# Attention and MLPs on one core: transposes and ranking one step later, and every second product with v moved out by ScalarE and added by GpSimd

## The chip, the cores and the metric

The kernel runs on one NeuronCore of a Trainium2 chip. The metric is the device time of one execution in microseconds, the median of several. Engines are named as in the profile: PE is TensorE (PEld its weight loads), DVE is VectorE, ACT is ScalarE, POOL is GpSimd, and SP issues most DMAs.

## What is computed

All in float32, and three stages in a row:

```
q_assign, k_assign = argmax over 16 centroids of the normalised q and k (per head)
scores = q @ k.T / 8, masked where q_assign != k_assign      16 heads of 768 x 64
x = softmax(scores) @ v                                      1536 tokens x 512
x = rational(x @ moe_w_in) @ moe_w_out                       d_ff 2048, P(h)/Q(h) elementwise
out = (silu(x @ w_gate) * (x @ w_val)) @ moe2_w_out          d_ff 1536
```

## The kernel before, in words

To keep float32 accuracy every operand is split into a high and a low part, so that a product is two or three matmuls (`three`, L1107 on; the names end in `_hi` and `_lo`). Each engine has its own program, written out in one block per engine, and they meet by semaphores.

The attention is a loop over `STEPS`. Step `s` holds the scores of tile `s` (96 tiles: 16 heads, 6 tiles of 128 queries each), and, so many steps behind, what follows for earlier tiles. On each engine the parts of a step run in the order in which they are written:

- PE: scores of tile `s` (L1226, L1229) into one of two double banks; transposes of the probabilities of tile `s - LAG` (L1239) into the two banks at `PT_BANK`, once DVE has read the tile before; a third of a product with v (L1254, L1256) into `O_BANK`; then, in some steps, the ranking's transposes (L1278), ranking (L1292) and centroid logits (L1313) of a head to come.
- DVE: cluster rows (L1024, L1026), `neg_max` of tile `s` (L1035), in steps divisible by 3 the row sums and reciprocals (L1046, L1049), `probT_lo` of tile `s - LAG` in two halves (L1057), `x_raw` (L1066), logit sum and maximum (L1072, L1074), `is_top` (L1080).
- ACT: exp of tile `s - 1` (L811), `topT` (L819), `probT_hi` in two halves (L829), `x_part` (L839), `logit_lo` (L861).
- POOL: normalising three tiles every third step (L589), splitting a head's q and k (L597 to L606) in steps divisible by 6, v (L614, L617) three steps later, the first MLP's weights (L624, L626), and every fourth product the x pair (L636, L638).

A product `g` is half a head: 384 query columns, summed over three steps. It begins `PV_LAG = LAG + 3` steps behind. Its result in `O_BANK` is two halves of 64 rows, which must be added: ACT copies one out to `x_part`, DVE adds the other to it into `x_raw`. The next product waits for that, since there is one bank. POOL splits `x_raw` of two heads into `x_hi` and `x_lo`, `X_STEP` steps behind.

The preparation of a head `h` (split, logits, sum, top, transposes, ranking, cluster rows: the stages `S_SPLIT` to `S_CLUSTER`) is placed by `head_at`, 18 steps ahead of the head's scores, and its rows go by SP's queue as small DMAs (`send_cluster`, L390) into `qk_low`, which the first score of the head waits for.

The first MLP begins inside the loop: PE makes the hidden values of tiles 0 to 3 in pieces in steps 96 to 103 (`TAIL_CHUNKS`), and ACT, DVE and POOL do tile 0 in step 98 and tile 1 in step 100 (`TAIL`; `hidden_read`, `mlps`, `mlp1`), ACT its second part in steps 99 and 101 (`TAIL_LOG`; `hidden_finish`). `mlps(1)` has six instructions of DVE (L925 to L953), and its last waits for `g_hi` of ACT's step 101. After the loop `first_result(0)` uses `O_BANK` and so waits for the last extraction. POOL's part of tile 2 (L516) stands behind the last x pair.

```
def pv_at(step):
    g, third = (step - PV_LAG) // HALF, (step - PV_LAG) % HALF
    return (g, third) if 0 <= g < NG else (None, None)
```

## Time and profile before

| | |
|---|---|
| runs | 794.30, 794.31, 795.95 us, median 794.31 |
| profiled execution | 794.28 us, its span 792.5 us |
| busy in the span | PE 781.2 (99%), PEld 697.7, DVE 571.9, ACT 517.3, POOL 522.7 us |
| HBM | 46 GB/s over the span |
| attention loop | 0 to about 263 us: x_part 32 times, from 37.0 to 262.2 us |

Rows of a timeline are: start in us from the span's start, duration, engine, line, operation, output<-inputs, shapes, count, and in brackets how long the engine sat idle before and what ended that. The end of a matmul is modelled, so that PE reads as busy in parts of its waits; the starts are measured.

### The profile page before, as it was taken

The numbers are of one execution on the slowest core, as the hardware profiler recorded it, in microseconds if no ns is written. First come the engines' busy times: TensorE is split into PE (matmuls) and PEld (weight loads), VectorE is DVE, ScalarE is ACT, GpSimd is POOL, SyncE is SP. The second block draws the span as 40 slices with busy tenths as digits, with TensorE's granted clock in tenths as the row PEclk, the third lists the DMA queues.
The fourth block names the chain that finished last, engine by engine and source line by source line (L and its number), as shares of the span: only waits on it lengthen the run. The fifth ranks groups of instructions, "written<-read, shape, count | busy, mean of one in ns | idle before, by whom it ended". The sixth has DMA issues, their size and how long they took to land.

```text
span 792.5 us, 12617 instructions
## 1 busy us (share of the span) xinstructions
PE 781.2 (99%) x4204; PEld 697.7 (88%) x4204; DVE 571.9 (72%) x1043; ACT 517.3 (65%) x957; POOL 522.7 (66%) x457
## 2 busy tenths in 40 slices
PE   8999999999999999999999999999999999999998
PEld 7799999999998888888888888899999999999997
DVE  5899999999997888778777777745445545554453
ACT  4888888888887787777767889744444444333322
POOL 4767988998575799322222288888889876655620
PEclk8999999999999999999999999999999999999999
DMA  8776555454310700000000011241111114111102
GB/s 206 180 199 162 143 140 125 116 145 121 85 60 19 221 28 0 1 1 1 1 1 0 1 55 54 66 147 50 32 54 53 37 45 134 54 28 53 28 1 80
DMA packets 57681, 57.92 MB, mean 73 GB/s; under 512 B 6608, under 2 KB 44304, under 8 KB 57616
## 3 DMA queue, kind: packets, MB, share of 16 engines
q1 hardware_dynamic: 57376, 56.52, 26.6%
q8 instruction: 34, 0.56, 0.3%
q10 hardware_dynamic: 240, 0.59, 0.3%
q14 instruction: 31, 0.25, 0.1%
HBM read 33.59 MB, written 3.15 MB: 46 GB/s over the span
## 4 chain that ended last, share of the span: by engine, by line
PE 87%; DVE 8%; issue 2%; ACT 2%; DMA 0%; DVEq 0%; ACTq 0%
PE ps L1111 18%; PE ps L1109 18%; PE ps L1110 18%; PE ps L1239 6%; PE ps L1204 4%; PE ps L1205 4%; PE ps L1203 4%; DVE neg_max L1035 3%; DVE probT_lo L1057 3%; PE ps L1254 3%; PE ps L1226 3%; PE ps L1256 3%; PE ps L1313 2%; PE ps L1229 2%; ACT prob L811 1%
## 5 line engine op out<-in xcount | busy, mean ns | idle before, releaser
L516 POOL TENSOR_TENSOR den<-den,mag 128x512 f32<-128x512 f32 x48 | 62.3, 1298 | 121.8 <-ACT den L689 121.6
L1111 PE MATMUL ps<-x_hi,w_lo 128*128 128x512 f32 (+1 forms) x384 | 139.5, 363 | 0.0
L1109 PE MATMUL ps<-x_hi,w_hi 128*128 128x512 f32 (+1 forms) x384 | 139.4, 363 | 0.0
L1110 PE MATMUL ps<-x_lo,w_hi 128*128 128x512 f32 (+1 forms) x384 | 139.3, 363 | 0.0
L575 POOL TENSOR_TENSOR w_lo<-w_raw,w_hi 128x768 fp32r<-128x768 f32 (+1 forms) x48 | 101.6, 2125 | 56.4 <-ACT w_hi L742 56.4
L589 POOL TENSOR_SCALAR prob<-prob,row_inv 128x768 f32<-128x768 f32 x96 | 85.6, 907 | 39.2 <-DVE row_inv L1049 38.7
L829 ACT ACTIVATE probT_hi<-ps 128x384 fp32r<-128x384 f32 x192 | 84.2, 489 | 25.9 <-PE ps L1239 24.2
L1057 DVE TENSOR_TENSOR probT_lo<-ps,probT_hi 128x384 fp32r<-128x384 f32 x192 | 96.8, 545 | 5.3 <-ACT probT_hi L829 4.0
L1035 DVE TENSOR_REDUCE neg_max<-ps 128x1 f32<-128x768 f32 x96 | 91.1, 950 | 8.8 <-PE ps L1229 8.5
L811 ACT ACTIVATE prob<-ps,neg_max 128x768 f32<-128x768 f32 x96 | 86.8, 905 | 10.8 <-DVE neg_max L1035 10.1
L1239 PE MATMUL ps<-ident,prob 128*128 128x128 f32 x576 | 81.7, 277 | 4.4 <-DVE probT_lo L1057 4.1
L1239 PEld LDWEIGHTS ps<-ident,prob 128*128 128x128 f32 x576 | 65.6, 140 | 17.0 <-issue 9.9
L1109 PEld LDWEIGHTS ps<-x_hi,w_hi 128*128 128x128 f32 x384 | 72.1, 188 | 8.2
L1110 PEld LDWEIGHTS ps<-x_lo,w_hi 128*128 128x128 f32 x384 | 72.1, 188 | 8.2
L1111 PEld LDWEIGHTS ps<-x_hi,w_lo 128*128 128x128 f32 x384 | 72.1, 188 | 7.5
L1111 PE MATMUL ps<-g_hi,w_lo 128*128 128x512 f32 x192 | 74.8, 390 | 0.0
L1110 PE MATMUL ps<-g_lo,w_hi 128*128 128x512 f32 x192 | 74.8, 390 | 0.0
L1109 PE MATMUL ps<-g_hi,w_hi 128*128 128x512 f32 x192 | 74.8, 390 | 0.0
L1254 PE MATMUL ps<-probT_hi,v_split 128*128 128x384 f32 x192 | 72.5, 378 | 0.0
L763 ACT ACTIVATE act_hi<-ps 128x384 fp32r<-128x384 f32 x48 | 23.6, 492 | 64.6 <-DVE ps L992 43.7
L1256 PE MATMUL ps<-probT_lo,v_split 128*128 128x384 f32 x192 | 64.6, 337 | 0.0
L959 DVE TENSOR_TENSOR sum<-ps,gate 128x384 f32<-128x384 f32 x24 | 13.4, 557 | 68.9 <-PE ps L1111 68.9
(145 smaller groups left out, 1987.5 us busy)
## 6 DMA issues: line engine op xcount, KB each, us to landing
k_hihi<-qk_hi SPq DMA_DIRECT2D x32, 192.0 KB, 4.0
w_raw<-in_moe_w_gate SPq DMA_DIRECT2D x48, 128.0 KB, 2.3
w_raw<-in_moe_w_val SPq DMA_DIRECT2D x48, 128.0 KB, 2.5
w_raw<-in_moe_w_in SPq DMA_DIRECT2D x16, 256.0 KB, 3.7
w_raw<-in_moe_w_out SPq DMA_DIRECT2D x16, 256.0 KB, 5.0
qk_raw<-in_q SPq DMA_DIRECT2D x16, 192.0 KB, 3.4
q_hilo<-qk_hi SPq DMA_DIRECT2D x16, 192.0 KB, 3.4
qk_low<-qk_hi SPq DMA_DIRECT2D x16, 192.0 KB, 4.5
```

Of the source, the lines that this page charges most:

```text
L575: did(g.tensor_tensor(lo[:, wave, :], raw[:, wave, :], hi[:, wave, :].bitcast(F32), ALU.subtract), s_w2lo)
L589: did(g.tensor_scalar(prob[i][:, :], prob[i][:, :], row_inv[:, i:i + 1], 1.0, ALU.mult, ALU.mult), s_norm)
L811: s.activation(prob[i % T][:, :].rearrange("p (c n) -> p c n", c=2), ps[:, bank:bank + 2, 0:HC], ACT.Exp, bias=neg_max[:, i % T:i % T + 1] ...
L829: s.activation(probT_hi[g % 2][:, n * HALF:(n + 1) * HALF, c:c + P], ps[:, PT_BANK + n, 0:HC].rearrange("p (k n) -> p k n", k=HALF), ACT.C ...
L1035: v_.tensor_reduce(neg_max[:, i % T:i % T + 1], ps[:, bank:bank + 2, 0:HC], AX.XY, ALU.max, negate=True).then_inc(s_max, 1)
L1057: v_.tensor_tensor(probT_lo[g % 2][:, keys, c:c + P], ps[:, PT_BANK + n, 0:HC].rearrange("p (k n) -> p k n", k=HALF), probT_hi[g % 2][:, k ...
L1109: mm(dst, hi, m_hi, start=start, stop=False)
L1110: mm(dst, hi, m_lo, start=False, stop=False)
L1111: return mm(dst, lo, m_hi, start=False, stop=stop)
L1239: last = transpose(ps[:, PT_BANK + n, kt % HALF * P:(kt % HALF + 1) * P], prob[i % T][:, kt * P:(kt + 1) * P], ident[:, :])
L1254: mm(ps[:, O_BANK, 0:HC], vv, probT_hi[g % 2][:, kt, :], start=(kt == 0), stop=False)
L1256: last = mm(ps[:, O_BANK, 0:HC], vv, probT_lo[g % 2][:, kt, :], start=False, stop=(kt == T - 1))
```

## The change

`LAG` goes from 5 to 6, so transposes, `probT_hi`, `probT_lo` and the products come one step later. The preparation stages from the logits on come one step later for heads 2 and up (head 2 had this already up to its sum). The x pairs of POOL follow their product by 1 step instead of 5 (the last one by 2).

The extraction of a product depends on its number now. Even ones go as before. For odd ones ACT copies both halves, one into `x_raw` and one into `x_low`, a tile that lies where `x_hi` will, DVE does nothing, and POOL adds the two (384 columns of both heads of a pair in one instruction) ahead of the split. PE waits for `s_xsum` or `s_xmain` by turns.

```
--- before.py
+++ after.py
@@ -85,6 +85,7 @@
     x_hi = at("x_hi", [P, DC, NTOK], F32R, X_AT)
     x_lo = at("x_lo", [P, DC, NTOK], F32R, X_AT + X_BYTES)
 
+    x_low = at("x_low", [P, DC, NTOK], F32, X_AT)
     x_raw = at("x_raw", [P, DC, NTOK], F32, X_AT + X_BYTES)
 
     w1_raw = [at(f"w1_raw{u}", [P, U1], F32, W_AT + u * 8 * U1) for u in range(NF1)]
@@ -218,8 +219,8 @@
     s_cen_in, s_par_in = sem("s_cen_in"), sem("s_par_in")
     s_qk_in = [sem(f"s_qk_in{i}") for i in range(3)]
     s_v_in = [sem(f"s_v_in{i}") for i in range(2)]
-    s_vhi, s_vlo, s_logit_lo, s_logit_sum, s_xpart, s_xsum = (sem(x) for x in (
-        "s_vhi", "s_vlo", "s_logit_lo", "s_logit_sum", "s_xpart", "s_xsum"))
+    s_vhi, s_vlo, s_logit_lo, s_logit_sum, s_xpart, s_xsum, s_xmain = (sem(x) for x in (
+        "s_vhi", "s_vlo", "s_logit_lo", "s_logit_sum", "s_xpart", "s_xsum", "s_xmain"))
     s_copy = [sem(f"s_copy{i}") for i in range(3)]
     s_clrows = [sem(f"s_clrows{i}") for i in range(3)]
     s_w1_in = [sem(f"s_w1_in{u}") for u in range(NF1)]
@@ -237,6 +238,7 @@
         "s_score", "s_max", "s_exp", "s_den", "s_inv", "s_norm"))
     s_pT, s_pT_hi, s_pT_lo, s_pv, s_xhi, s_xlo = (sem(x) for x in (
         "s_pT", "s_pT_hi", "s_pT_lo", "s_pv", "s_xhi", "s_xlo"))
+    s_xboth = sem("s_xboth")
     s_w1p_hi, s_w1p, s_w1hi, s_w1lo = (sem(x) for x in ("s_w1p_hi", "s_w1p", "s_w1hi", "s_w1lo"))
     s_w2sum, s_w2hi, s_w2lo, s_wohi, s_wolo = (sem(x) for x in (
         "s_w2sum", "s_w2hi", "s_w2lo", "s_wohi", "s_wolo"))
@@ -254,10 +256,10 @@
 
     R_LAG = 3
     COPIES, CLROWS = 16 * 6, 16 * T
-    LAG = 5
+    LAG = 6
     PV_LAG = LAG + HALF
     V_STEP = 3
-    X_STEP, LAST_X_STEP = 5, 2
+    X_STEP = 1
     PREP_LEAD = 18
     FIRST_STEP = -PREP_LEAD
     S_SPLIT, S_CEN, S_LOGIT, S_SUM, S_TOP, S_TOPT, S_RANK, S_CLUSTER = 0, 2, 6, 8, 9, 10, 11, 12
@@ -269,7 +271,9 @@
 
 
         for h in range(NH):
-            late = -4 * (h == 1) + (h == 2 and stage <= S_SUM)
+            late = -4 * (h == 1)
+            if h >= 2:
+                late = 1 if stage >= S_LOGIT else int(h == 2)
             if T * h + late == step + PREP_LEAD - stage:
                 return h
         return None
@@ -626,13 +630,14 @@
                     did(g.tensor_tensor(w1_lo[u][:, :], w1_raw[u][:, :], w1_hi[u][:, :].bitcast(F32),
                                     ALU.subtract), s_w1p)
                 g1, third = pv_at(step - X_STEP)
-                if pv_at(step - LAST_X_STEP) == (NG - 1, HALF - 1):
-                    g1, third = NG - 1, HALF - 1
                 if third == HALF - 1 and g1 % 4 == 3:
-                    pool.wait_ge(s_xsum, g1 + 1)
+                    h = g1 // 2
+                    pool.wait_ge(s_xmain, h + 1)
+                    pool.wait_ge(s_xsum, h + 1)
                     finish_last()
-                    h = g1 // 2
                     xh, xl, raw = x_pair(x_hi, h), x_pair(x_lo, h), x_pair(x_raw, h)
+                    did(g.tensor_tensor(raw[:, HC:S], raw[:, HC:S], x_pair(x_low, h)[:, HC:S], ALU.add), s_xboth)
+                    finish_last()
                     did(g.tensor_scalar(xh, raw, 1.0, 1.0, ALU.mult, ALU.mult), s_xhi)
                     pool.wait_ge(s_xhi, h // 2 + 1)
                     did(g.tensor_tensor(xl, raw, xh.bitcast(F32), ALU.subtract), s_xlo)
@@ -834,10 +839,14 @@
                 if third == HALF - 1:
                     r = (g // 2) % 2 * D
                     sc.wait_ge(s_pv, g + 1)
-                    if g:
-                        sc.wait_ge(s_xsum, g)
-                    s.activation(x_part[r:r + D, :], ps[D - r:P - r, O_BANK, 0:HC], ACT.Copy
-                                 ).then_inc(s_xpart, 1)
+                    if g % 2 == 0:
+                        if g:
+                            sc.wait_ge(s_xsum, g // 2)
+                        s.activation(x_part[r:r + D, :], ps[D - r:P - r, O_BANK, 0:HC], ACT.Copy
+                                     ).then_inc(s_xpart, 1)
+                    else:
+                        s.activation(x_of(x_low, g), ps[D - r:P - r, O_BANK, 0:HC], ACT.Copy)
+                        s.activation(x_of(x_raw, g), ps[r:r + D, O_BANK, 0:HC], ACT.Copy).then_inc(s_xmain, 1)
                 if head_at(step, S_CEN) == 0:
 
                     sc.wait_ge(s_cen_t, 4)
@@ -1059,9 +1068,9 @@
                                          probT_hi[g % 2][:, keys, c:c + P].bitcast(F32),
                                          ALU.subtract).then_inc(s_pT_lo, 1)
                 g, third = pv_at(step)
-                if third == HALF - 1:
-
-                    ve.wait_ge(s_xpart, g + 1)
+                if third == HALF - 1 and g % 2 == 0:
+
+                    ve.wait_ge(s_xpart, g // 2 + 1)
                     r = (g // 2) % 2 * D
                     v_.tensor_tensor(x_of(x_raw, g), ps[r:r + D, O_BANK, 0:HC],
                                      x_part[r:r + D, :], ALU.add).then_inc(s_xsum, 1)
@@ -1142,7 +1151,8 @@
                 pe.wait_ge(s_glo, n + 1)
                 if n == 0:
                     pe.wait_ge(s_pT_lo, 2 * NT)
-                    pe.wait_ge(s_xsum, NG)
+                    pe.wait_ge(s_xsum, NH)
+                    pe.wait_ge(s_xmain, NH)
                 for d in range(DC):
                     if u == 0 and n:
                         pe.wait_ge(s_yraw, (n // NF1 - 1) * DC + d + 1)
@@ -1248,7 +1258,7 @@
                         pe.wait_ge(s_pT_lo, T * (g + 1))
                         pe.wait_ge(s_vlo, h + 1)
                         if g:
-                            pe.wait_ge(s_xsum, g)
+                            pe.wait_ge(s_xsum if g % 2 else s_xmain, (g + 1) // 2)
                     for kt in (2 * third, 2 * third + 1):
                         vv = v_split[h % 2][:, kt, :, :].rearrange("p two d -> p (two d)")
                         mm(ps[:, O_BANK, 0:HC], vv, probT_hi[g % 2][:, kt, :], start=(kt == 0),
```

## Rows read from the trace of the kernel before

**Rows 1.** Busy time by stretch: span, then PE, PEld, DVE, ACT, POOL, clock, DMA.
```profile
46.80:213.00 166.20, 162.75 (x1116) 153.17 (x1114) 157.78 (x334) 138.84 (x317) 139.21 (x139) 1.00 0.54 135
213.00:243.00 30.00, 29.45 (x192) 26.95 (x189) 29.46 (x57) 26.73 (x61) 22.72 (x24) 1.00 0.15 46
...
263.40:520.00 256.60, 256.60 (x1142) 213.71 (x1142) 197.73 (x289) 196.76 (x303) 140.24 (x101) 1.00 0.10 30
```

**Rows 2.** What PE waited for, whole span: us in total, times, longest.
```profile
PE ps L1239 <- DVE probT_lo L1057: 4.1, 14, 0.5
```

**Rows 3.** One head, DVE in order of time: start, us, line, operation.
```profile
134.25 0.96 DVE L1035 TENSOR_REDUCE neg_max<-ps 128x1 f32<-128x768 f32 x1 [0.31 <-PE ps L1229]
...
136.05 0.36 DVE L1072 TENSOR_TENSOR ps<-ps,logit_lo 128x192 f32<-128x192 f32 x1
...
137.58 0.15 DVE L1046 TENSOR_REDUCE row_den<-row_sum 128x3 f32<-128x6 f32 x1
...
140.93 0.56 DVE L1066 TENSOR_TENSOR x_raw<-ps,x_part 64x384 f32<-64x384 f32 x1
...
142.51 1.02 DVE L1057 TENSOR_TENSOR probT_lo<-ps,probT_hi 128x384 fp32r<-128x384 f32 x2
```

**Rows 4.** The same head, PE.
```profile
138.53 0.92 PE L1239 MATMUL ps<-ident,prob 128*128 128x128 f32 x6 [0.21 <-DVE probT_lo L1057]
...
141.64 0.41 PE L1254 MATMUL ps<-probT_hi,v_split 128*128 128x384 f32 x1
```

**Rows 5.** The same head, ACT.
```profile
132.87 0.49 ACT L839 ACTIVATE x_part<-ps 64x384 f32<-64x384 f32 x1 [0.16 <-PE ps L1256]
133.38 0.90 ACT L811 ACTIVATE prob<-ps,neg_max 128x768 f32<-128x768 f32 x1
...
134.58 0.88 ACT L829 ACTIVATE probT_hi<-ps 128x384 fp32r<-128x384 f32 x2 [0.20 <-PE ps L1239]
```

**Rows 6.** Groups by line, 0 to 300 us: a two-input operation of POOL.
```profile
L617 POOL TENSOR_TENSOR v_split<-v_raw,v_split 128x384 fp32r<-128x384 f32 x16 | 16.2, 1013 | 1.3
```

**Rows 7.** The last two cluster-row DMAs of head 2, their landing, and PE's next score.
```profile
L390 SPq DMA_DIRECT2D qk_low<-clusterT x2: 592/593/594, 36.4 to 37.1; - x2
...
DMA to landing us min/median/max: 1.9/2.0/2.1
...
39.20 0.52 PE L1226 MATMUL ps<-k_hihi,q_hilo 128*128 128x384 f32 x2
```

**Rows 8.** End of attention, ACT.
```profile
247.45 0.49 ACT L839 ACTIVATE x_part<-ps 64x384 f32<-64x384 f32 x1 [0.16 <-PE ps L1256]
...
249.92 0.61 ACT L685 ACTIVATE mag<-ps 128x512 f32<-128x512 f32 x1
...
262.18 0.48 ACT L839 ACTIVATE x_part<-ps 64x384 f32<-64x384 f32 x1 [0.98 <-PE ps L1256]
```

**Rows 9.** End of attention, DVE.
```profile
252.07 0.69 DVE L944 TENSOR_TENSOR num<-num,ps 128x512 f32<-128x512 f32 x1 [1.36 <-ACT num L693]
...
253.46 1.01 DVE L1057 TENSOR_TENSOR probT_lo<-ps,probT_hi 128x384 fp32r<-128x384 f32 x2
...
256.92 0.69 DVE L925 SCALAR_TENSOR_TENSOR den<-den,ps 128x512 f32<-128x512 f32 x1
...
260.42 0.68 DVE L953 TENSOR_TENSOR g_lo<-ps,g_hi 128x512 fp32r<-128x512 f32 x1
```

**Rows 10.** End of attention, PE.
```profile
251.39 0.82 PE L1239 MATMUL ps<-ident,prob 128*128 128x128 f32 x6
...
254.15 0.92 PE L1239 MATMUL ps<-ident,prob 128*128 128x128 f32 x6
...
257.04 0.41 PE L1254 MATMUL ps<-probT_hi,v_split 128*128 128x384 f32 x1
...
263.41 0.47 PE L1109 MATMUL ps<-g_hi,w_hi 128*128 128x512 f32 x1
```

**Rows 11.** End of attention, POOL.
```profile
266.20 1.29 POOL L516 TENSOR_TENSOR den<-den,mag 128x512 f32<-128x512 f32 x1
```

More of the change, by code:

```diff
@@ L256, in build_program @@
     COPIES, CLROWS = 16 * 6, 16 * T
-    LAG = 5
+    LAG = 6
     PV_LAG = LAG + HALF
     V_STEP = 3
-    X_STEP, LAST_X_STEP = 5, 2
+    X_STEP = 1
     PREP_LEAD = 18
@@ L271, in head_at @@
         for h in range(NH):
-            late = -4 * (h == 1) + (h == 2 and stage <= S_SUM)
+            late = -4 * (h == 1)
+            if h >= 2:
+                late = 1 if stage >= S_LOGIT else int(h == 2)
             if T * h + late == step + PREP_LEAD - stage:
@@ L1061, in _ @@
                 g, third = pv_at(step)
-                if third == HALF - 1:
-                    ve.wait_ge(s_xpart, g + 1)
+                if third == HALF - 1 and g % 2 == 0:
+                    ve.wait_ge(s_xpart, g // 2 + 1)
                     r = (g // 2) % 2 * D
```

32 lines of the change are left out of this document (20 added, 12 removed).

## Prediction

> **What bounds the kernel now.** I read the busy times by stretch first. In the MLPs TensorE is busy for all of 256.6 us out of 256.6 [rows 1], so a microsecond lost ahead of them is not won back there; the end moves by as much. In the attention loop four engines are near full: from 46.8 to 213 us PE 162.8, DVE 157.8, ACT and POOL 139 of 166.2 us [rows 1]. Which of PE and DVE sets the pace is read from PE's waits: only one kind recurs, the transposes of L1239 waiting for probT_lo, 14 times, 4.1 us in all, at most 0.5 [rows 2]. So PE sets the pace, with about one stop per head of 6 steps. The busy PE records hide part of each (their ends are modelled), so I take 0.53, near the longest, rather than the mean of 0.3: 0.38 at the transposes and 0.15 at a product (both below). A lighter DVE can then return at most 0.53 x 13 = 6.9 us in the loop, for the 13 heads prepared in it.
>
> **Where the stop per head comes from.** DVE meets PE at 134.25, where neg_max has waited for its score [rows 3]. From there DVE works without a pause: logit sum and maximum (136.05), row sums and reciprocal (137.58), is_top, three neg_max, three pairs of probT_lo, and at 140.93 x_raw of the even product, which ends at 141.49 [rows 3]. PE is stopped by this chain twice [rows 4]: the transposes at 138.53 waited for probT_lo (0.21 by the row, nearer 0.4 by the starts around it), and the product at 141.64 begins 0.15 after x_raw ended; it needs the same bank.
>
> **The change in the loop.** Three things move by one step together: the transposes (LAG), the ranking stages from the logits on, and with LAG the products. Relative to each other they stand as before: the logit sum is still two steps ahead of the even product's extraction. What is removed is x_raw of the odd product. It lies one step ahead of the logit sum, beside two long steps of PE with logits, and DVE has 0.31 us idle behind it before 134.25 [rows 3]. Taking it away makes that idle time longer; the chain from 134.25 to 141.49 keeps every member, for the row sums (steps divisible by 3, not moved) are in it once before and once after. **Removed DVE work, 16 instructions of 0.55 us: worth 0 in these heads.**
>
> The row sums of the second half do move against the rest. They stood in a long logit step; now they follow the even extraction directly, in the short step with the ranking. There x_raw ends at 141.49, one neg_max of 0.96 follows, and probT_lo starts at 142.51 [rows 3], which leaves nothing between them. Row sums and reciprocal add 0.27 (0.15 for the first and about as much for the second), less the 0.1 by which neighbours on DVE overlap: probT_lo 0.15 later, and the next transposes with it; in heads where probT_lo waits for ACT anyway, about 0.04. **I take 0.1 x 13 = +1.3 us; bounds 0 and 2.3.**
>
> ScalarE gets a second copy of 0.49 us per head. Before, x_part at 132.87 is followed by exp at 133.38 and probT_hi at 134.58, 0.2 us after the engine was free [rows 5]. Two like copies take 0.88, so they start 0.4 apart [rows 5]; exp moves by 0.42, and the first probT_hi runs from 134.8 to 135.3 instead of to 135.07. DVE is through with neg_max at 135.1 to 135.2 [rows 3]; but the row sums now stand ahead of probT_lo in just this step, so DVE comes at 135.39. Hidden, with 0.03 us to spare: **0, bounds 0 and 1.3.** If that cover were gone the price would be a rival below. For PE the bank comes free after 2 copies (0.9) instead of copy plus x_raw (1.1): 0.
>
> GpSimd adds 8 two-input operations on 128x384, each 1.01 as its like [rows 6], 8.1 us into 139.2 busy of 166.2 [rows 1]. The x pair moves from the step with a head's split to the one with v_split, the smaller of the two, and the norms have one step more before their transposes. SP's queue waits on GpSimd's v_split, which still stands ahead of the x pair: 0. The GpSimd page of the Trainium skill (GPSIMD Engine Reference, section Engine selection) says to keep elementwise adds off this engine, at about twice the vector engine's time. Here 1.01 against 0.55 bears out the ratio; were they on the path that ends last, the 8 adds would cost 3.7 us by it, which I do not count since POOL has that time.
>
> **The start.** With transposes one step later, PE and DVE have less to do ahead of step 12: one step's transposes and one step's products, about 1.4 us of PE (a step without extras is some 2.1: a third each for scores, transposes and products, and two of these three are missing once). But step 12 opens head 2, whose cluster rows are sent by SP. The last two go out at 36.4 and 37.1 and land 1.9 to 2.1 us later, at 39.2, and the score starts at 39.20 [rows 7]. SP issues them one after another behind other copies of the same queue, whose own conditions the change leaves alone, so they come no earlier. PE is ready 1.4 sooner, at about 37.8, and waits. **Start: +0.1 us; the 1.4 us of work that left here is lost, as it comes back at the end.** Bounds -1.3 (the rows are not what ends it) and +0.3.
>
> **The last steps with scores** (213 to 243 us): no ranking, short steps, DVE busy 29.5 of 30.0 [rows 1]. Here a dropped x_raw helps; but the two copies of ACT now delay exp and so probT_hi, about 0.5 us in each of 2 places, and step 96 waits 0.2 more since the even extraction falls just before it. **0, bounds -1.0 and +0.9.**
>
> **The end of attention: the main term.** The MLP's first two tiles are begun at steps 98 and 100 (TAIL), and these did not move with LAG. Each engine runs its steps in order.
> (a) Step 98: ACT now first does the two copies of product 29 (before: nothing). Its last copy of this kind was at 247.45 and a step is 254.15-251.39 = 2.76 us [rows 8, 10], so they start at 250.2 and end at 251.1; mag of tile 0 moves from 249.92 [rows 8] to 251.1, 1.2 later. DVE's num (252.07) waits for it, probT_lo (253.46) stands behind num [rows 9], and the transposes at 254.15 start 0.15 after its first half ended [rows 10]: no slack. **+1.2 us.**
> (b) Step 100: DVE does tile 1's six instructions, from 256.92 to 261.10 [rows 9], 4.2 us. Before, the last probT_lo and x_raw of product 30 stood ahead of them and PE's product at 257.04 followed at once. Now both are of step 101, behind them. With (a), the transposes of step 100 are at 255.4, the probT_lo of that step ends 2.1 later at 257.5, the block runs to 261.7, then probT_lo 0.93 and x_raw 0.56 to 263.2, 0.15 to PE: 263.3. PE is through with step 101 at 255.4 + 2 x 2.76 = 260.9. **+2.3 us.**
> (c) The last product is now at step 104, behind the last chunk. Before, x_part (262.18) and x_raw ran beside the chunk of step 103 and first_result began at 263.41 [rows 8, 10]. Now nothing covers 0.2 + 2 copies 0.9 + 0.15. **+1.2 us.**
> (d) The extra step's transposes and products, 1.3 us, are the work that left the start. **+1.3 us.**
> GpSimd's last pair takes 1.0 longer, which moves den at 266.20 [rows 11] by 1.0 against PE; tile 2's g_lo then comes about 0.1 ahead of its use: 0, at most 0.3.
> Together +6.0; bounds 3.5 and 7.5.
>
> **Sum.** 0.1 + 1.3 + 0 + 6.0 = 7.4 us on the profiled execution's 794.28, whose span is 792.5; that execution is within 0.03 of the median 794.31. Forecast **801.6**; its own range, with the ends of the terms not all at once, 798 to 804.5.
>
> **Rivals.**
> *Faster: DVE is the true bound.* Busy 95% in the loop [rows 1], it stops PE 14 times [rows 2]. If the stops go in all 13 heads (-6.9), the row sums cost nothing, the start keeps its work (-1.3) and the last scores gain (-1.0), the time is 794.3+6.0-9.2 = 791.1, give or take 2. Against it: the chain of rows 3 loses no member. A rule of the Trainium skill (Perfetto Trace Analysis, Identifying the Most-Contended Engine) judges TensorE's room by weight-load time. That is 153.2 of 166.2 us here [rows 1], 13 us of room against the 4 to 7 that the waits allow; by it the time could come to 781, and it has 0.02 of this rival's chance. Chance 0.14, of it 0.04 within the bound of no change.
> *No change.* The end is absorbed: (a) and (b) overlap with other slack, and only 1 to 2 us stay, against a small gain in the loop: 793 to 796. For it: DVE has idle time there, 1.36 us ahead of 252.07 [rows 9]. Chance 0.07.
> *Slower still: ACT's second copy is not covered.* It decides from 0.03 us of lateness of probT_hi in the step of rows 5. If DVE would be there at once, probT_hi holds it by the whole 0.42: 0.4 x 13 = 5.2 on top, 806.8. Chance 0.07.
> *The change doesn't do what it says.* The bank's waits are split over two semaphores and each product has its own; I see no case where the old path stays. 0.
> Forecast: 0.72.
>
> **Numbers.** A difference under 0.2% (1.6 us) can't be told from no change. Forecast and last rival give slower, 0.79, and 0.01 of the no-change case does, 0.8 together; same is 0.04 of that case and 0.04 of the faster one, 0.08; faster is the rest, 0.12. The range 796.5 to 804.5 holds the forecast's range and 1.5 us towards no change, where most of what I may have overrated at the end would put it.
>
> **What would show it.** Right: the waits of L1239 for probT_lo still about 13, of 0.3 to 0.6, a step later; x_raw of DVE 16 times with an idle DVE where the other 16 were; PE gaps near 254, 261 and 268 us of about 1.2, 2.3 and 1.2; first_result's start at 269 to 271 instead of 263.41; PE busy without gaps behind it. PE's clock stays at its 2.4 GHz level, as in the stretches of rows 1. Wrong: fewer than 6 waits of L1239 on probT_lo, the score of step 12 before 38.5, or no PE gap over 1 us between 250 and 275.

## The result, and the profile after

The kernel with the change took 802.84 us (median of 6 runs, 801.08 to 803.57) beside 795.13 us for the kernel before (794.23 to 797.3) on the same chip. The ratio is 1.009, with a 95% interval of 1.0071 to 1.0108: slower by 0.9%. The forecast was 801.6, within 796.5 to 804.5.

The profiled execution took 801.45 us, 7.17 more than before; its span is 799.7. Busy time by stretch, same columns as [rows 1]:

```profile
46.14:213.00 166.86, 164.89 (x1114) 152.52 (x1114) 149.51 (x320) 142.26 (x329) 144.23 (x144) 1.00 0.53 135
```

DVE has 8.3 us less to do in the loop (157.8 to 149.5), ACT 3.4 and POOL 5.0 more. The loop is not shorter. What DVE did with its 8 us stands in one group of the kernel after, columns as in [rows 6] (the last part is the idle time ahead of the group):

```profile
L1044 DVE TENSOR_REDUCE neg_max<-ps 128x1 f32<-128x768 f32 x96 | 91.2, 951 | 20.4 <-PE ps L1239 20.0
```

and in the same group of the kernel before:

```profile
L1035 DVE TENSOR_REDUCE neg_max<-ps 128x1 f32<-128x768 f32 x96 | 91.1, 950 | 8.8 <-PE ps L1229 8.5
```

The window is 0 to 300 us. DVE waits 11.6 us longer ahead of `neg_max`: the removed additions became idle time there. x_raw itself is down to 16 additions from 32.

**Where the 7 us are.** PE's first matmul of a step is the score; here is that of steps 0, 6 and 81 before (step 12 is in [rows 7]), and of steps 0, 6, 12 and 81 after:

```profile
15.62 0.56 PE L1226 MATMUL ps<-k_hihi,q_hilo 128*128 128x384 f32 x2
...
25.28 0.51 PE L1226 MATMUL ps<-k_hihi,q_hilo 128*128 128x384 f32 x2
...
209.07 0.51 PE L1226 MATMUL ps<-k_hihi,q_hilo 128*128 128x384 f32 x2
```

```profile
15.54 0.56 PE L1236 MATMUL ps<-k_hihi,q_hilo 128*128 128x384 f32 x2
...
24.32 0.59 PE L1236 MATMUL ps<-k_hihi,q_hilo 128*128 128x384 f32 x2 [0.42 <-ACT prob L816]
...
38.48 0.59 PE L1236 MATMUL ps<-k_hihi,q_hilo 128*128 128x384 f32 x2 [0.69 <-issue]
...
209.56 0.60 PE L1236 MATMUL ps<-k_hihi,q_hilo 128*128 128x384 f32 x2
...
270.53 0.47 PE L1118 MATMUL ps<-g_hi,w_hi 128*128 128x512 f32 x1 [1.16 <-ACT x_raw L849]
```

The last row is `first_result`, which was at 263.41 [rows 10]. The stretches between such starts make the table that the rest of this text uses (us; "steps 39 to 75" are six heads from the middle of the loop, six times a steady head):

| kernel (profiled execution) | step 0 at | 0 to 6 | 6 to 12 | 12 to 27 | 27 to 81 | of it 39 to 75 | 81 to 95 | median of runs |
|---|---|---|---|---|---|---|---|---|
| before | 15.62 | 9.66 | 13.93 | 37.11 | 132.76 | 88.40 | 31.15 | 795.13 |
| after | 15.54 | 8.78 | 14.16 | 37.55 | 133.53 | 88.91 | 31.76 | 802.84 |
| tail_late | 17.47 | 8.76 | 13.61 | 37.62 | 133.53 | 88.89 | 31.78 | 797.43 |
| dve_adds | 15.59 | 8.80 | 13.86 | 38.13 | 133.99 | 89.27 | 31.72 | 802.68 |
| copies_only | 15.26 | 11.76 | 13.77 | 37.15 | 135.47 | 90.08 | 31.83 | 799.23 |
| sums_late | 15.44 | 8.48 | 14.73 | 37.92 | 133.13 | 88.61 | 31.91 | 803.05 |
| rows_first | 14.31 | 8.81 | 13.24 | 37.66 | 133.55 | 88.93 | 31.81 | 796.75 |
| rank_old | 15.30 | 9.78 | 13.64 | 38.66 | 139.59 | 93.05 | 33.02 | 806.09 |
| rank_old_sums | 15.02 | 10.08 | 13.55 | 38.00 | 136.66 | 91.13 | 32.30 | 801.77 |
| swap | 15.36 | 8.74 | 14.01 | 37.83 | 135.81 | 90.53 | 32.08 | 800.61 |
| rank_later | 15.17 | 9.39 | 13.29 | 38.86 | 134.08 | 89.26 | 32.43 | 799.32 |
| before_rank_later | 16.11 | 11.94 | 14.41 | 38.05 | 134.08 | 89.30 | 31.09 | 798.78 |
| sums_apart | 14.27 | 8.98 | 13.21 | 40.73 | 133.03 | 88.05 | 31.49 | 799.44 |
| before_rows | 17.48 | 9.69 | 13.92 | 37.12 | 132.83 | 88.46 | 31.18 | 796.02 |

After against before: step 0 starts within 0.08 us of the same time; steps 0 to 6 take 0.88 less; steps 6 to 27 cost 0.67, 27 to 81 cost 0.77, 81 to 95 cost 0.61, and from step 95 on (263.41 - 240.22 = 23.19 before, 270.53 - 241.32 = 29.21 after) 6.02. The sum, -0.08 - 0.88 + 0.67 + 0.77 + 0.61 + 6.02 = 7.11, is the later start of `first_result` within rounding. From there to the end of the span are 529.1 us before and 529.2 after.

The 0.88 us won ahead of step 6 come with the change and not by chance. Before, PE stood once for `is_top` of head 2, in step 4; this row of its list of waits is missing after, where that head's maximum, `is_top` and its transposes are one step later:

```profile
PE ps L1278 <- DVE is_top L1080: 1.2, 1, 1.2
```

All kernels with LAG 6 and the ranking moved take 8.48 to 9.39 us from step 0 to 6. The kernels with that wait take 9.66 (before), 9.69, 9.78 and 10.08 (the last two, rank_old and rank_old_sums, have LAG 6 as well), and two more of them, copies_only and before_rank_later, 11.76 and 11.94, with PE's clock down for some 3 us there (see the last section).

**The end of attention**, PE after. Three starts stand apart from the matmul before them. Without a wait the next matmul starts 0.23 us after one of 512 columns and 0.18 after one of 384:

```profile
254.94 0.40 PE L1120 MATMUL ps<-x_hi,w_lo 128*128 128x512 f32 x1
256.34 0.92 PE L1249 MATMUL ps<-ident,prob 128*128 128x128 f32 x6 [1.00 <-DVE probT_lo L1066]
...
261.71 0.40 PE L1120 MATMUL ps<-x_hi,w_lo 128*128 128x512 f32 x1
264.25 0.41 PE L1264 MATMUL ps<-probT_hi,v_split 128*128 128x384 f32 x1 [2.15 <-DVE x_raw L1075]
...
269.03 0.34 PE L1266 MATMUL ps<-probT_lo,v_split 128*128 128x384 f32 x1
```

They are 1.40, 2.54 and 1.50 from start to start, so PE lost 1.2, 2.3 and 1.3 there. The other two engines show what each waited for; ACT:

```profile
251.75 0.48 ACT L849 ACTIVATE x_raw<-ps 64x384 f32<-64x384 f32 x1
252.13 0.58 ACT L690 ACTIVATE mag<-ps 128x512 f32<-128x512 f32 x1
...
269.90 0.49 ACT L849 ACTIVATE x_raw<-ps 64x384 f32<-64x384 f32 x1
```

and DVE:

```profile
254.26 0.69 DVE L953 TENSOR_TENSOR num<-num,ps 128x512 f32<-128x512 f32 x1 [2.50 <-ACT num L698]
...
255.65 1.01 DVE L1066 TENSOR_TENSOR probT_lo<-ps,probT_hi 128x384 fp32r<-128x384 f32 x2
...
258.36 0.68 DVE L934 SCALAR_TENSOR_TENSOR den<-den,ps 128x512 f32<-128x512 f32 x1
...
263.54 0.56 DVE L1075 TENSOR_TENSOR x_raw<-ps,x_part 64x384 f32<-64x384 f32 x1
```

The two copies push `mag` of tile 0 from 249.92 [rows 8] to 252.13, DVE's num waits for it and holds probT_lo; six instructions of the MLP, from 258.36 on, stand ahead of the last x_raw; and the last copy, at 269.90, is all that `first_result` waits for.

**The loop.** PE's waits for probT_lo, whole span, after:

```profile
PE ps L1249 <- DVE probT_lo L1066: 1.7, 4, 1.0
```

Only 4 waits for probT_lo, against 14 in [rows 2]; yet six heads take 88.91 us instead of 88.40. The stops are there in the starts and too short for this view. In one head, DVE and then PE:

```profile
144.57 0.16 DVE L1055 TENSOR_REDUCE row_den<-row_sum 128x3 f32<-128x6 f32 x1
...
144.85 0.99 DVE L1066 TENSOR_TENSOR probT_lo<-ps,probT_hi 128x384 fp32r<-128x384 f32 x2
```

```profile
144.94 0.52 PE L1239 MATMUL ps<-qk_low 80*128 80x384 f32 x2
145.53 0.92 PE L1249 MATMUL ps<-ident,prob 128*128 128x128 f32 x6
...
148.01 0.52 PE L1239 MATMUL ps<-qk_low 80*128 80x384 f32 x2
148.37 0.82 PE L1249 MATMUL ps<-ident,prob 128*128 128x128 f32 x6
```

Undisturbed, transposes follow the second score by 0.36 (148.01 to 148.37); at 145.53 they follow by 0.59, behind a probT_lo that stands behind the row sums. No wait is printed beside it.

The old stop, once per head in the step with `is_top`, is still there and shorter. From the second score to the transposes were 0.72 and 0.84 us by turns before and are 0.65 in each head after, against the undisturbed 0.36: a stop of 0.29 instead of 0.36 and 0.48.

**The last scores.** Steps 88, 91 and 94 take 2.52 us each, against 2.09, 2.06 and 2.06 before. In step 91, DVE and then PE:

```profile
232.07 0.16 DVE L1055 TENSOR_REDUCE row_den<-row_sum 128x3 f32<-128x6 f32 x1
```

```profile
233.03 0.92 PE L1249 MATMUL ps<-ident,prob 128*128 128x128 f32 x6 [0.19 <-DVE probT_lo L1066]
```

Here too the row sums stand just ahead of the probT_lo (232.36) that PE waits for; the extraction is now in the step before them and not two steps before.

### The profile page after: what moved, and what is told of

It reads as the page before. It is cut to its first block, busy times and chain, and to the rows that moved or that the text cites. A ratio compares the mean times of both kernels' runs of the same rounds, so it can differ in the third digit from the quotient of the medians.

```text
span 799.7 us, 12610 instructions
## 1 busy us (share of the span) xinstructions
PE 785.0 (98%) x4204; PEld 696.7 (87%) x4204; DVE 561.8 (70%) x1027; ACT 522.5 (65%) x973; POOL 531.3 (66%) x465
## 4 chain that ended last, share of the span: by engine, by line
PE 91%; DVE 5%; issue 2%; ACT 1%; DMA 0%; DVEq 0%; ACTq 0%
PE ps L1118 18%; PE ps L1120 18%; PE ps L1119 18%; PE ps L1249 7%; PE ps L1214 4%; PE ps L1215 4%; PE ps L1213 4%; PE ps L1236 4%; PE ps L1264 3%; PE ps L1239 3%; PE ps L1266 3%; PE ps L1323 3%; DVE probT_lo L1066 2%; DVE neg_max L1044 2%; PE ps L1288 0%
```

## The experiments

Three kernels start from the kernel before (copies_only, before_rank_later, before_rows), all others from the kernel after.

### tail_late: the MLP's first tiles one step later

```diff
-    TAIL_CHUNKS = {NT + n: ((2 * n) // DC, (2 * n) % DC) for n in range(AHEAD * DC // 2)}
-    TAIL = {NT + 2: 0, NT + 4: 1}
-    TAIL_LOG = {NT + 3: 0, NT + 5: 1}
+    TAIL_CHUNKS = {NT + 1 + n: ((2 * n) // DC, (2 * n) % DC) for n in range(AHEAD * DC // 2)}
+    TAIL = {NT + 3: 0, NT + 5: 1}
+    TAIL_LOG = {NT + 4: 0, NT + 6: 1}
```

> The changed kernel with the MLP's first two tiles and PE's hidden-value pieces one step later too (97 to 104 instead of 96 to 103, tiles 0 and 1 in steps 99 and 101), so that they stand to the transposes as before the change. Theory (the end of attention is the main term): the gaps of PE of 1.40, 2.55 and 1.50 us between transposes, products and first_result go, step 96 becomes a light step that costs some 0.3 to 0.8; the time is 3.5 to 5 us under the changed kernel, 2.5 to 4 over the kernel before. Rival (the loop or the start lost the time): within 1 us of the changed kernel, about 7.5 over before.

Measured: 797.43 us (10 runs), ratio to before 1.003 (1.002 to 1.004), 5.4 us below the kernel after. The three places in its trace, PE:

```profile
258.51 0.40 PE L1120 MATMUL ps<-x_hi,w_lo 128*128 128x512 f32 x1
258.78 0.92 PE L1249 MATMUL ps<-ident,prob 128*128 128x128 f32 x6
...
261.39 0.40 PE L1120 MATMUL ps<-x_hi,w_lo 128*128 128x512 f32 x1
261.66 0.41 PE L1264 MATMUL ps<-probT_hi,v_split 128*128 128x384 f32 x1
...
267.99 0.40 PE L1118 MATMUL ps<-g_hi,w_hi 128*128 128x512 f32 x1
```

The starts follow each other by 0.27 and 0.27 where the kernel after had 1.40 and 2.54, and `first_result` waits for nothing. From step 95 to it (242.77 to 267.99) are 25.22 us, 4.0 less than after. The theory's place is right and its size a little small: 5.4 below the kernel after where 3.5 to 5 was expected, 2.3 over before where it was 2.5 to 4. Of the other 1.4 in the medians, the traces have 0.55 in steps 6 to 12. The rest may be clock: in sums_late PE's granted clock falls behind the stop of 2.1 us, which costs 1.5 us (see there). Of the six runs of the kernel after, the three with a mean clock of 0.993 or 0.994 took 802.66 to 803.06, while the profiled one, without this loss, took 801.45 at 0.996; dve_adds took 803.46 and 803.48 at 0.993 and 0.994, 801.79 and 801.91 at 0.996. But one run of the kernel after at 0.996 took 803.57, so this is likely and not shown. Most of the change's loss is thus the edit that was not made with it: tiles placed by absolute step numbers while the products moved.

### dve_adds: the move without the copies

Every product is extracted as in the kernel before; LAG, ranking and x pairs stay as in the kernel after.

```diff
-                    if g % 2 == 0:
-                        if g:
-                            sc.wait_ge(s_xsum, g // 2)
-                        s.activation(x_part[r:r + D, :], ...)
-                    else:
-                        s.activation(x_of(x_low, g), ps[D - r:P - r, O_BANK, 0:HC], ACT.Copy)
-                        s.activation(x_of(x_raw, g), ps[r:r + D, O_BANK, 0:HC], ACT.Copy).then_inc(s_xmain, 1)
+                    if g:
+                        sc.wait_ge(s_xsum, g)
+                    s.activation(x_part[r:r + D, :], ...)
...
-                if third == HALF - 1 and g % 2 == 0:
+                if third == HALF - 1:
```

> The changed kernel with every product extracted as the even ones (one copy of ScalarE, the add by VectorE, no add of GpSimd): only the later transposes and ranking and the moved x pairs are left. Theory: the dropped DVE adds were worth nothing in the heads and the second copy cost nothing there, so only step 98 gains (one copy ahead of tile 0 instead of two, 0.4 us) and the last scores change by up to 0.5 either way: 0 to 1 us under the changed kernel, 6.5 to 8 over before. Rival (DVE relief pays): 4 us or more over the changed kernel. Rival (ACT's second copy is what costs): 3 us or more under it.

Measured: 802.68 us (4 runs), ratio 1.0091 (1.0073 to 1.011), not to be told from the kernel after. In the loop it can be: six heads take 89.27, against 88.91 with the copies and 88.40 before, and kernels with the same loop agree within 0.06 (88.40 and 88.46; 88.91, 88.89 and 88.93). So the move costs 0.87 / 6 = 0.14 us per head, and the copies give 0.06 back. By the place in the head, the move's price lies in the step behind the ranking (2.98 us in every second head instead of 2.73), and what the copies give back in the step ahead of `is_top` (2.12 us in every second head instead of 2.25). Steps 81 to 95 take 31.72 with the additions on DVE and 31.76 with the copies: the longer last scores come from the move.

### copies_only: the copies without the move

The kernel before, with the odd products copied by ACT and added by POOL, LAG 5, the old ranking steps and the old steps of the x pairs.

> The kernel before with only the new extraction of odd products (two copies of ScalarE, add of GpSimd), LAG 5, old ranking, old x pairs. Theory: here the row sums do not stand ahead of probT_lo in the step behind the copies, so probT_hi, 0.24 us late, delays probT_lo and with it the whole chain to the even x_raw: 0.24 x 13 = 3 us in the heads, the end of attention unchanged: 2 to 4 us over before. Rival (the copy is covered anyway): within 1 us of before. Rival (DVE relief pays): 3 us or more under before.

Measured: 799.23 us (7 runs), ratio 1.0043 (1.003 to 1.0055): 4.1 us slower than before. That is next to the 2 to 4 expected, but by another cause: the theory had it from a late probT_hi. PE's waits for its transposes:

```profile
PE ps L1249 <- DVE probT_lo L1066: 4.0, 14, 0.5
PE ps L1249 <- POOL prob L591: 2.5, 5, 0.5
```

POOL and one of PE's stops, one head:

```profile
139.32 1.00 POOL L639 TENSOR_TENSOR x_raw<-x_raw,x_low 128x384 f32<-128x384 f32 x1
...
143.27 2.67 POOL L591 TENSOR_SCALAR prob<-prob,row_inv 128x768 f32<-128x768 f32 x3
```

```profile
144.23 0.87 PE L1249 MATMUL ps<-ident,prob 128*128 128x128 f32 x6 [0.54 <-POOL prob L591]
```

The 14 waits for probT_lo are all still there: taking the odd x_raw from DVE returned nothing in this placement. What is new is GpSimd: with the addition ahead of it, the x pair ends 1 us later, the normalising behind it too, and with LAG 5 the transposes come just then. The later x pair and the extra step of LAG in the change are what makes room for the addition. ACT's second copy cost next to nothing: the step in which it delays exp takes 2.16 and 2.20 us by turns (before 2.14 and 2.16). exp starts 0.38 later behind the copies, but probT_hi then follows it by 0.87 where it was 1.20 (ACT had waited 0.20 for PE, [rows 5]), so that probT_hi comes 0.39 behind the start of `neg_max` instead of 0.33, still before DVE is through with it. From step 27 to 95 this kernel loses 3.4 us; 2.1 more of its profiled execution went ahead of step 6, where PE's clock was low for 3.3 us (last section).

The rule of the Trainium skill against elementwise adds on this engine (GPSIMD Engine Reference, Engine selection) is borne out here as far as the engines go: 1.00 us on POOL for 128x384, where DVE needs 1.01 for two operations of that shape (probT_lo), and it lies on the path. But one such addition takes the place of two of DVE's 64x384 at 0.55 each, since it covers both heads of a pair; as a sum of work the move is even.

### sums_late: row sums one step later

```diff
-                if (step - HALF) % HALF == 0 and 0 <= (step - HALF) // HALF < NG:
+                if (step - HALF - 1) % HALF == 0 and 0 <= (step - HALF - 1) // HALF < NG:
```

> The changed kernel with the row sums and reciprocals (and so the normalising) one step later on DVE, where they stood relative to the ranking before the change. Theory: the stop at the transposes behind the ranking step (about 0.24 in every second head) goes, -1.3 us, but the cover of probT_hi in the step behind the two copies goes too, +0.24 x 13 = +3: 1 to 2.5 us over the changed kernel. Rival (the row sums' new place is the whole loss of the loop and nothing is covered by it): 1 to 1.5 us under the changed kernel.

Measured: 803.05 us (4 runs), ratio 1.01 (1.0075 to 1.0125). That is neither the 1 to 2.5 us over the kernel after of the theory nor the rival's 1 to 1.5 under it. Six heads take 88.61, so 0.05 us less per head than after, but steps 6 to 27 are 0.9 longer and the end from step 95 on 1.5: no gain. The 1.5 are the clock's. PE stops for 2.14 us as in the kernel after, and from its start at 264.55 to 267.7 the granted clock is 0.50, the 1.2 GHz level (columns as in [rows 1]):

```profile
265.00:267.00 2.00, 2.00 (x7) 1.81 (x7) 1.57 (x3) 0.00 (x0) 0.00 (x0) 0.50 0.83 279
```

In the kernel after the clock is 1.00 behind the same stop. The row sums left the step ahead of the ranking step, and the ranking step behind it went from 2.99 to 2.73 us in every second head. They landed ahead of probT_lo in the step with is_top, and the step behind that one grew by 0.10 and 0.24 by turns. (Step lengths are means of the distance between score starts, by place in two heads, over steps 42 to 77.)

### rows_first and before_rows: the start

SP sends head 2's cluster rows ahead of the v load and the k_hi copy; rows_first on tail_late, before_rows on the kernel before.

```diff
+            send_cluster(2)
             load_v(2)
             for h in range(3, NH + 1):
...
-                send_cluster(h - 1)
+                if h > 3:
+                    send_cluster(h - 1)
```

> The kernel with the change and with the MLP's first tiles one step later (as tail_late, 797.4), in which SP sends head 2's cluster rows ahead of its v load and k_hi copy. Theory (at the start PE waits for these rows, so the work that LAG took from there is lost): step 12's score starts 1.0 to 1.4 us sooner than it otherwise would, and the time is 796.2 (795.8 to 796.6). Rival (the rows are not what ends it): no change, 797.4.

Measured: 796.75 us (12 runs), ratio 1.0022 (1.0012 to 1.0032). SP issues the six rows from 27.30 on; in the kernel after it was from 32.41 on. SP's queue of the one and of the other:

```profile
27.30 5.01 SPq L394 DMA_DIRECT2D qk_low<-clusterT  x6
```

```profile
32.41 4.71 SPq L394 DMA_DIRECT2D qk_low<-clusterT  x6
```

Step 12 then starts at 36.36 with no wait beside it. From step 6 to 12 it takes 13.24 us; the kernels with LAG 6 and the old order take 13.55 to 14.73, and the waits printed at step 12 go from none to 1.07. So the wait is real, 0.3 to 1.5 us in one execution or another, and it is not given back later (12 to 27: 37.66 beside 37.55 and 37.62). Against its parent tail_late it is 0.4 in the traces (13.24 beside 13.61), where 1.0 to 1.4 was expected. In the medians rows_first is 0.7 below tail_late, 0.5 less than I expected and just outside the range given, and the two intervals overlap.

> The kernel before, with SP sending head 2's cluster rows ahead of its v load and k_hi copy. Theory (with LAG 5 TensorE comes to step 12 about when these rows land, so it does not wait for them; only with LAG 6 it does): 794.6 +- 0.4, no change; the score of step 12 stays about 13.9 us behind that of step 6. Rival (the rows hold up the start before as well): 1 us or more less, 793.6 or below.

Measured: 796.02 us (12 runs), ratio 1.0009 (0.9997 to 1.0021): no difference that the runs can tell, as expected, though the median lies above the 794.6 +- 0.4 given. The rows go out at 29.71 to 33.6 instead of 33.7 to 37.7, and step 6 to 12 takes 13.92, before 13.93. With LAG 5 PE does not wait for them; only LAG 6 has something to win.

### rank_old, rank_old_sums and swap: where the copies may stand

rank_old is tail_late with the ranking stages back at their old steps (`late = -4 * (h == 1) + (h == 2 and stage <= S_SUM)`); rank_old_sums adds the edit of sums_late.

> As tail_late, with the ranking stages of heads 2 and up back at their old steps, so that the ranking step no longer directly follows the step with the row sums. Theory (the row sums behind the even extraction in the ranking step are what the loop lost): 0.2 to 0.3 us less per head, 13 heads, 794.2 (793.5 to 795.2). Rival (the placement of the ranking has no price, the loop's loss is from the two copies): 797.4 +- 0.4. Second rival (v_split, normalising or x pair of GpSimd now collide with the logits): 799 or more, with PE waiting for POOL's prob.

> As rank_old, with DVE's row sums one step later too, out of the step in which DVE does logit sum and maximum. Theory (the row sums are a link of the chain from neg_max to probT_lo): 0.2 us less per head than rank_old, 791.5 (790.5 to 793). Rival (what is gained in one step is lost where they land, as in sums_late): as rank_old, 794.2. Second rival (GpSimd's normalising comes late by it): 796 or more, PE waiting for POOL's prob.

Measured: 806.09 us (4 runs), ratio 1.0137 (1.0123 to 1.0151), and 801.77 us (5 runs), ratio 1.0091 (1.0075 to 1.0106). I had expected 794.2 and 791.5; both were wrong, and so was the thought behind them. The second rival of rank_old (799 or more) had the size but not the cause: PE waits 18 times for probT_lo, 9.4 us in all, and not for GpSimd's prob. rank_old, ACT and DVE:

```profile
124.64 0.48 ACT L847 ACTIVATE x_raw<-ps 64x384 f32<-64x384 f32 x1
125.14 0.33 ACT L868 ACTIVATE logit_lo<-ps 128x192 f32<-128x192 f32 x1
```

```profile
125.51 0.37 DVE L1079 TENSOR_TENSOR ps<-ps,logit_lo 128x192 f32<-128x192 f32 x1 [0.84 <-ACT logit_lo L868]
```

The odd product's two copies now share a step with logit_lo, DVE's logit sum waits 0.84 us for it, and neg_max, probT_lo and PE's transposes stand behind that wait: 0.6 us at the transposes as printed (0.8 by the starts), and 93.05 us for six heads. PE's row:

```profile
128.00 0.92 PE L1247 MATMUL ps<-ident,prob 128*128 128x128 f32 x6 [0.61 <-DVE probT_lo L1064]
```

rank_old_sums takes a member out of that same chain and wins 0.32 per head (93.05 to 91.13), more than the 0.2 expected, on a path that had become longer.

swap is tail_late with even products copied by ACT and odd ones added by DVE.

> As tail_late, with the roles of the products exchanged: even ones by two copies of ACT and GpSimd's add, odd ones by ACT and DVE. Theory (of the two extractions by DVE, the even one stands in the chain that stops PE, the odd one beside idle time, so the change dropped the wrong one): 0.1 to 0.2 us less per head, 795.8 (795.0 to 796.6). Rival (DVE's work is worth the same wherever it lies): 797.4 +- 0.4.

Measured: 800.61 us (6 runs), ratio 1.0069 (1.0057 to 1.0082), instead of 795.8: wrong in sign. PE in the step with the ranking:

```profile
145.15 0.34 PE L1266 MATMUL ps<-probT_lo,v_split 128*128 128x384 f32 x1
145.56 0.39 PE L1302 MATMUL ps<-topT,rank 128*128 128x256 f32 x1
```

The ranking starts 0.41 after the product's last matmul, where the kernel after has 0.18: ACT makes topT behind the two copies. The step with the ranking is 0.19 us longer than in tail_late, the head 0.27. Of the 0.27, 0.06 is the price of the odd addition on DVE, as in dve_adds. In rank_old the head is 0.69 longer ((93.05 - 88.89) / 6), but no run has LAG 6 with the ranking at its old place and single copies, so the second copy's own share of it is not shown. Together the two runs suggest why the ranking moved with LAG. In a head of six steps ACT has two steps in which a second copy delays a small tile that others wait for (logit_lo, topT). The change keeps the odd product's copies one step ahead of logit_lo, and that needs the ranking to move when the products do.

### rank_later and before_rank_later: the ranking another step later

```diff
-                late = 1 if stage >= S_LOGIT else int(h == 2)
+                late = (1 if h == 2 else 2) if stage >= S_LOGIT else int(h == 2)
```

> As rows_first (796.75), with the ranking stages from the logits on one more step later for heads 3 and up (logits on TensorE in steps 2 and 3 of 6, logit sum in step 4, ranking behind the step that follows the row sums). Theory: DVE's chain starts where it last has idle time, behind TensorE's last step with logits; the first row sums (0.3 us) then lie in front of that point, the ranking's long step no longer directly follows row sums, and logit_lo and topT of ACT stay clear of the two copies. So TensorE's stop per head shrinks by 0.2 to 0.4 us: 792.5 (791 to 794.5), and the waits for probT_lo in the loop go. Rival (logit sum and maximum now lie directly ahead of the even extraction, so that chain gets tighter and what is gained is lost there, as in sums_late): 796.75 or up to 3 more.

> The kernel before, with one edit: the ranking stages from the logits on one step later for heads 3 and up. Theory: with LAG 5 the logit sum then shares its step with the row sums and lies directly ahead of the even extraction's step; the chain keeps all its members and starts 1 step later, so the stop per head moves but stays: 794.6 +- 1.5. Rival (what the loop gains in rank_later comes from the place of the ranking alone, LAG has no part in it): 3 us or more below before, 791.5.

Measured: 799.32 us (6 runs), ratio 1.0052 (1.0033 to 1.0071), and 798.78 us (9 runs), ratio 1.0035 (1.002 to 1.005). For rank_later the rival was right. In the step with is_top, which is one step later now, the transposes follow the score by 0.46 us instead of 0.65, so this stop shrank by 0.19; but the product behind them waits for x_raw, the ranking step's transposes stop too (0.51 and 0.63 by turns, undisturbed 0.35), and the step with is_top takes 2.64 and 2.78 us instead of 2.59. rank_later, DVE and PE:

```profile
129.52 0.54 DVE L1077 TENSOR_TENSOR x_raw<-ps,x_part 64x384 f32<-64x384 f32 x1
```

```profile
129.28 0.92 PE L1251 MATMUL ps<-ident,prob 128*128 128x128 f32 x6
130.20 0.41 PE L1266 MATMUL ps<-probT_hi,v_split 128*128 128x384 f32 x1
```

The product starts 0.92 behind the transposes (1.06 in every second head), where the kernel after has 0.68 in this step and 0.57 in undisturbed ones. Half of the trace's loss against rows_first (1.2 of 2.35 us, steps 12 to 27) is a single stop in step 26: three operations of DVE on the parameters of P and Q, placed by absolute step (`step == 4 * T`), take 1.8 us there (71.43 to 73.18; in rows_first 0.8, with no stop behind them), `neg_max` and probT_lo stand behind them, and PE's transposes at 74.66 wait 1.03 us. In before_rank_later the same place opens to 0.92 and 1.06. Neither number that I gave for it was met (794.6 +- 1.5, or 791.5): the placement before is the better one of the two.

### sums_apart: only the row sums that moved against the rest

As rows_first; the row sums of odd halves two steps later, those of even halves where they were.

```diff
-                if (step - HALF) % HALF == 0 and 0 <= (step - HALF) // HALF < NG:
-                    half = (step - HALF) // HALF
+                half = next((b for b in range(NG) if step == HALF * (b + 1) + 2 * (b % 2)), None)
+                if half is not None:
```

> As rows_first (796.75), with only the second row sums of each head (those in the step between the even extraction and the ranking step, the ones that moved against the rest) two steps later, where DVE waits 0.5 us for TensorE anyway. Theory (the step ahead of the ranking step lost 0.07 and 0.25 us by turns to these sums, 0.16 on average, and they cost nothing where DVE is idle): 0.16 x 13 = 2.1 us less, 794.7 (794.0 to 795.5). Rival (what is gained is lost again further on): 796.75 +- 0.5. Second rival (GpSimd's normalising, blocked 1.7 us longer, comes late): 798 or more.

Measured: 799.44 us (5 runs), ratio 1.0057 (1.0042 to 1.0071), not 794.7. The trace holds both answers. In the steady loop six heads take 88.05 instead of 88.93: 0.15 per head, the price expected, and less than the 88.40 of the kernel before. But steps 12 to 27 take 40.73 instead of 37.66. GpSimd's queue in the early heads:

```profile
43.78 2.67 POOL L595 TENSOR_SCALAR prob<-prob,row_inv 128x768 f32<-128x768 f32 x3 [3.59 <-DVE row_inv L1059]
...
48.25 1.83 POOL L612 TENSOR_TENSOR qk_lo<-qk_raw,qk_hi 128x768 fp32r<-128x768 f32 x1
```

and PE soon after:

```profile
53.38 0.59 PE L1237 MATMUL ps<-k_hihi,q_hilo 128*128 128x384 f32 x2 [2.08 <-issue]
```

The normalising waits 3.59 us for row_inv with the split of a head behind it; qk_lo starts 3.6 later than in rows_first (44.64), and PE stops for 2.1 us before a head's first scores. That step costs 1.8 us against rows_first, and the two steps behind it 1.5 more: PE's granted clock is 0.50 from 55 to 58 us. I read this as the head's copies coming late by the split; the trace names no releaser at 53.38. A version that moves these row sums only from the fourth head on was not tried.

## Why the prediction was right, point by point

| term | forecast | measured |
|---|---|---|
| end of attention | +6.0 (3.5 to 7.5) | +6.02 |
| its three gaps | 1.2, 2.3, 1.2 | 1.2, 2.3, 1.3 |
| loop | +1.3 (0 to 2.3), 0.1 per head | 0.085 per head, +0.77 in 9 heads; steps 12 to 27 +0.44 |
| start | +0.1 (-1.3 to 0.3) | -0.65: steps 0 to 6 -0.88, 6 to 12 +0.23; step 0 itself -0.08 |
| last scores | 0 (-1.0 to 0.9) | +0.61 |
| sum on the profiled execution | +7.4 | +7.17 |

The main term is right in mechanism and size. That the sum is right to 0.3 us is in part luck: the start came 0.75 lower than forecast and the last scores 0.61 higher, and the two cancel. (7.4 on 794.31 is also 801.7 and not 801.6.)

**The end.** Right in size and in all three places. Step (a) was forecast to put mag at 251.1; it came at 252.13, since the whole end had moved by about 1.1 (loop, start and last scores), and the difference, 1.1, is near the 1.2 forecast. tail_late shows the mechanism by taking it away. What the forecast had no term for is PE's clock behind the 2.3 us of (b): it stayed at its 2.4 GHz level in the profiled execution, as forecast, and fell in that of sums_late at the same stop, for 1.5 us. The median of the runs, 802.84, is 1.2 above the forecast, and this may be part of it.

**The loop: the dropped additions "worth 0".** Right as far as PE's stops go: copies_only keeps 14 waits of 4.0 us. Slightly wrong in the new placement, where dve_adds shows that the copies return 0.06 us per head. **The row sums, +0.1 per head.** Right in cause, mis-sized: sums_apart measures them at 0.15 per head. The forecast's reason (neighbour of the even extraction) holds, with the price in the step that follows, 2.99 us instead of 2.73 in every second head. Too small by 0.05 and without the 0.06 from the copies, the two errors cancel: 0.15 - 0.06 = 0.09, measured 0.085. The size of this term is therefore partly luck.

**ACT's second copy "hidden, with 0.03 us to spare".** The outcome is right, the reading of the row was not. The forecast put probT_hi 0.22 later (134.8 instead of 134.58). In copies_only and in the kernel after it comes only 0.06 and 0.05 later against `neg_max`, since part of the time between exp and probT_hi in [rows 5] was ACT's wait for PE, which the copy fills. So the row sums were not needed as cover, as copies_only shows, where they do not stand in that step. What this copy can cost lies in two places that I did not look at, since the change leaves them free, logit_lo (rank_old) and topT (swap); their placements cost 0.69 and 0.27 us per head, in which the copy's own share was not measured alone.

**POOL's additions "0".** Right here, and not in general: with LAG 5 and the old steps of the x pairs they stop PE (copies_only). The 3.7 us set against them compared 8 additions of POOL with 8 of DVE, but they replace 16; 8 x 1.01 against 16 x 0.55 is no more work.

**The start.** Right that PE waits at step 12 for rows that SP sends, and rows_first and before_rows show that this holds with LAG 6 and not with LAG 5. The step that failed is "they come no earlier" than 39.2. PE's wait of 1.2 us for head 2's `is_top`, in step 4, went with the later ranking of that head, which the sum did not count; SP issued the rows from 32.41 instead of 33.69 on, and the score of step 12 came at 38.48. The term measures -0.65 instead of +0.1, within its bounds. What frees SP's queue sooner was not followed further.

**The last scores, 0.** Mis-sized by 0.61, within its bounds: the gain from a dropped x_raw was taken to balance two late exps and step 96. By dve_adds the copies as a whole change 0.04 us there, and the move has the rest. In steps 88, 91 and 94 transposes wait behind the row sums, a price that the forecast saw in the loop and left out here; moving half of these row sums gives back 0.32 us (sums_apart, 31.49 beside 31.81). The other half is not settled by a run.

**The signs.** Two of the three signs set for "wrong" came up though the forecast held: fewer than 6 waits for probT_lo (4 were listed), and step 12 before 38.5 (38.48). The second is the failed step of the start. The first was badly chosen. The recurring stop shrank to 0.29 us and the new one is 0.23, and stops of that size no longer print as waits, while the starts still show them; I had noted that busy PE records hide part of a wait and then counted waits all the same. Of the signs for "right", the places and sizes of the three gaps, `first_result` at 270.53, and the 16 x_raw of DVE held.

**The rivals.** DVE as the bound in the sense of that rival fell: 8.3 us less of its work, and 11.6 us more of its waiting. The absorbed end of "no change" fell with the three gaps. The uncovered copy (806.8) did not come about. By the weight-load time (Perfetto Trace Analysis, section Identifying the Most-Contended Engine, in the Trainium skill) PE would have room in the loop; PEld is at 152.5 of 166.9 us now, and the kernels run here found almost nothing of it: the best steady head, 88.05 / 6 = 14.68 us (sums_apart), is 0.06 below the 88.40 / 6 = 14.73 of the kernel before. They do not show that it can't be had.

No kernel that was run beats the one before. The best with LAG 6, rows_first, is 0.2% behind it.

## What to carry to other kernels

When a stage is shifted, list everything that was placed by an absolute step beside it; here two tiles of the next phase, left where they were, made 4.0 (by the traces) to 5.4 us (by the medians) of a loss of 7.7, and in rank_later three small operations at one fixed step made 1.2 of 2.35. Work taken from an engine that is 95% busy is worth what stands in the chain that stops the pacing engine, which may be nothing; price each instruction by where it lies, on the engine that gives it up and on the one that takes it, including the small tiles queued behind it there. And read a stop of a few tenths from the starts of the pacing engine, over several periods, before and after: lists of waits lose it. Where a stretch is longer without a new wait, look at the granted clock of that stretch before giving it a cause.

## What the runs showed of the hardware

The start moves by microseconds without an edit ahead of it: step 0 began at 15.62 in the kernel before and at 17.48 in before_rows, whose edit acts later, and over all profiled executions at 14.27 to 17.48. Sums of stretches have to begin behind it.

A stop of PE can cost more than its length, and the same stop does not always do so. Behind the 2.14 us at 264.55 in sums_late the granted clock was 0.50, its 1.2 GHz level, until 267.7, and the end of attention took 1.5 us more; behind 2.15 us at the same place in the kernel after it stayed 1.00. Behind the wait of 1.2 us for `is_top` in step 4 it fell to 0.5 for some 3 us in copies_only (23.3 to 26.6) and before_rank_later (24.8 to 28.1), and not in the kernel before or before_rows; steps 0 to 6 took 11.76 and 11.94 us in the first two, 9.66 and 9.69 in the others. In sums_apart it was 0.50 from 55 to 58 us, 1.6 us after a stop of 2.1 had ended at 53.38.

And two stops of the same kind differ in what the profile says of them: at 138.53 in the kernel before a start that is late by about 0.4 is printed as a wait of 0.21 [rows 4], at 145.53 in the kernel after one of 0.23 is not printed at all.
